# GpSimd fills in a pair's block sums before it halves the next pair's columns; one throwaway product; a later down matrix request

## The reference

```python
B, H, S, D = q.shape          # 4, 8, 768, 64
block, window = (32, 16)
nb = S // block               # 24
k_sum = k.reshape(B, H, nb, block, D).max(axis=3)
v_sum = v.reshape(B, H, nb, block, D).mean(axis=3)
scores_l = scale * np.matmul(q, k.transpose(0, 1, 3, 2))
mask_l = np.abs(pos[:, None] - pos[None, :]) < window
scores_s = scale * np.einsum('bhsd,bhnd->bhsn', q, k_sum) + np.log(block)
a = softmax(concat(where(mask_l, scores_l, -1e9), scores_s))
out = a @ concat(v, v_sum)
```

## Time and profile before

| | |
|---|---|
| median of 3 runs | 364.32 us (363.89, 364.32, 366.35) |
| the profiled execution | 365.38 us, of which its span is 363.5 us |
| PE busy | 326.4 us (90%), 3264 instructions |
| DVE busy | 172.5 us (47%) |
| ACT busy | 148.4 us (41%) |
| POOL busy | 101.0 us (28%) |
| DMA | 81.64 MB, 225 GB/s mean |
| mean granted TensorE clock | 0.974 |

### The profile page before, as it was taken

The page is one execution under the profiler, slowest core; times in us unless marked ns, Lnnn a source line. Parts: engine busy times, 40 slices in busy tenths (PEclk is TensorE's granted clock), DMA queues, the critical chain, the costliest instruction groups (busy, mean ns, idle before and its releaser), DMA issues.

```text
span 363.5 us, 9091 instructions
## 1 busy us (share of the span) xinstructions
PE 326.4 (90%) x3264; PEld 235.2 (65%) x3265; DVE 172.5 (47%) x391; ACT 148.4 (41%) x344; POOL 101.0 (28%) x181
## 2 busy tenths in 40 slices
PE   0869899999999899989867799999999999999993
PEld 0557677767666763323327248888888888888882
DVE  2546777878777562560114678423231323222331
ACT  1456778778778532221110073223132222313131
POOL 5466576676754300000000000222121212121211
PEclk9978999999999999999996799999999999999998
DMA  7999999999999996999950920110101101110101
GB/s 302 358 422 417 418 346 352 375 358 349 362 413 418 434 392 250 384 403 437 400 227 2 357 107 3 58 58 29 58 29 58 50 37 46 40 58 29 58 31 61
DMA packets 15147, 81.64 MB, mean 225 GB/s; under 512 B 2312, under 2 KB 2312, under 8 KB 10512
## 3 DMA queue, kind: packets, MB, share of 16 engines
q1 hardware_dynamic: 11936, 73.08, 50.7%
q0 software_dynamic: 1920, 6.29, 4.5%
q10 hardware_dynamic: 1264, 1.92, 1.6%
HBM read 74.99 MB, written 6.29 MB: 224 GB/s over the span
## 4 chain that ended last, share of the span: by engine, by line
PE 67%; DMA 11%; DVE 7%; ACT 7%; issue 4%; SPq 2%; POOL 1%; DVEq 0%; ACTq 0%; POOLq 0%
PE ps L923 35%; DMA ring<-in_moe_w 7%; PE ps L642 6%; DMA ring<-in_vt 4%; PE ps L619 3%; DVE ps L1187 3%; ACT work L990 3%; PE ps L655 3%; PE ps L909 3%; PE ps L628 2%; PE ps L761 2%; PE ps L611 2%; ACT work L1005 2%; SPq L296 2%; PE ps L810 2%
## 5 line engine op out<-in xcount | busy, mean ns | idle before, releaser
L923 PE MATMUL ps<-high_w2b,hid_high 128*128 (+1 forms) x184 | 71.7, 390 | 0.0
L923 PE MATMUL ps<-low_w2b,hid_high 128*128 (+1 forms) x184 | 71.7, 390 | 0.0
L923 PE MATMUL ps<-high_w2b,hid_low 128*128 (+1 forms) x184 | 71.6, 389 | 0.0
L990 ACT ACTIVATE work<-ps,small 128x120 f32<-128x120 f32 x192 | 53.6, 362 | 33.8 <-DVE small L1191 33.2
L576 POOL DMA_INDIRECT out_x<-work,small x24 | 23.6, 981 | 143.3 <-DVE small L1414 88.0
L1421 DVE SCALAR_TENSOR_TENSOR hid_low<-ps,hid_high 128x1024 fp32r<-128x1024 f32 x26 | 31.8, 1224 | 57.3 <-ACT hid_high L1102 57.2
L1084 ACT ACTIVATE work<-ps,small 128x512 f32<-128x512 f32 x24 | 16.5, 689 | 94.7 <-PE ps L923 87.8
L642 PE MATMUL ps<-ring,work 121*64 121x65 f32 x768 | 34.5, 232 | 8.8 <-ACT work L1005 4.0
L642 PEld LDWEIGHTS ps<-ring,work 121*64 121x64 f32 x768 | 27.8, 141 | 18.7 <-issue 11.3
L923 PEld LDWEIGHTS ps<-high_w2b,hid_low 128*128 128x128 f32 x184 | 34.6, 188 | 7.3
L923 PEld LDWEIGHTS ps<-high_w2b,hid_high 128*128 128x128 f32 x184 | 34.6, 188 | 6.8
(11 more groups left out here) (231 smaller groups left out, 363.6 us busy)
## 6 DMA issues: line engine op xcount, KB each, us to landing
ring<-in_moe_w SPq DMA_DIRECT2D x12, 2048.0 KB, 16.2
ring<-in_qk SPq DMA_DIRECT2D x16, 1104.0 KB, 8.5
ring<-in_v SPq DMA_DIRECT2D x16, 780.0 KB, 6.5
ring<-in_moe_w SPq DMA_DIRECT2D x10, 512.0 KB, 18.4
x_or_g<-in_moe_w SPq DMA_DIRECT2D x2, 2048.0 KB, 9.5
ring<-in_vt SPq DMA_DIRECT2D x7, 384.0 KB, 5.5
comb<-in_vt SPq DMA_DIRECT2D x7, 384.0 KB, 5.6
whole_w2b<-in_moe_w SPq DMA_DIRECT2D x4, 512.0 KB, 9.1
```

Of the source, the lines that this page charges most:

```text
L923: last = pe.matmul(ps[:, 4 + u, :], hidden_part[:, u, m * P:(m + 1) * P], matrix[:, bass.ds(e * UNIT + m * DM, DM)], start=m == 0 and i == ...
L990: act.activation(probs[u][:, j, :], sc[u][:, j // 2, (j % 2) * KC:(j % 2 + 1) * KC], ACT.Exp, bias=negmax[u][:, j:j + 1], scale=float(D) * ...
```

## The change

Three edits, and no transfer and no GpSimd instruction more or less:

```diff
@@ SP: request of the first expert's down matrix
             with sp.If(n_used < FEW + 1):
+                sp.wait_ge(w1b_part[0], 16)
                 for c in range(4):
@@ GpSimd: the loop over the pairs
             for n in range(1, B * NPAIR):
                 fill_gaps(n)
+                fill_sums(n)
                 if n + 1 < B * NPAIR:
                     halve(n + 1)
-                fill_sums(n)
@@ TensorE: the last round of the soft mixture's down product
                 for m in range(4):
                     if pr == E // 2 - 1 and m % 2 == 0:
+                        if m:
+                            keep_at_work(1, 1, comb[:, 0:BANK // SLOTS, :].rearrange("p q s -> p (q s)"))
                         for u in range(2):
                             pe.wait_ge(last_half[m // 2][u], 32)
```

## The result

| | before | changed |
|---|---|---|
| median | 364.11 us (4 runs) | 399.77 us (4 runs, 399.39 to 400.97) |
| ratio | | 1.0985, 95% interval 1.0947 to 1.1022 |
| span of the profiled execution | 363.5 us | 399.1 us |
| mean granted clock | 0.974 | 0.938 |

The account below looks back on a forecast made before the run. Attention was taken as bound by latency, a chain hopping between engines. Loop +31.0, clock +3.7, product -0.3 and request -0.4 make +34.0 us, taking the median 364.3 to 398.3 us; range 392 to 404.

Parts of the forecast that it names:

- The loop of 9.06 us, +31.0: Attention: the moved halving enters a loop of 9.06 us a pair against 6.41, paid over 14 turns, +31.0 us.
- The clock, +3.7: TensorE in attention: longer waits lower the clock in five of 14 turns, +3.7 us; bounds 0 to 10.4 us.
- two never follow each other: Attention: a slow pair leaves a shorter wait behind it, so two slow pairs in a row were not expected.
- After pair 15 nothing is moved.: From the last attention pair on, the new order was to add no time.
- The product, -0.3: Throwaway product in TensorE's 2.26 us wait for the last weights: fits for free, gains only by clock, -0.3 us.
- the request, -0.4: Down matrix requested after the up matrix's first part: gain at most 0.67 us, loss at most 1, taken as -0.4.
- Full clock with both small gains whole: Lower end of the prediction's own case: the loop without clock falls, product and request gains whole, 394.0 us.
- TensorE's fourteen waits behind pair 1: Sign in attention: TensorE waits for GpSimd ahead of each pair's first product, 14 times, over 30 us in all.
- R2: Later attention gives expert weights more time, winning back up to 25 us, down to 373 us; 4%.
- R1: Attention: the next pair's first product has time in hand, so the late halving is free, about 361 us; 3%.
- R3: The clock stays low throughout attention, making TensorE the bound: up to +84 us, 448 us; 3%.
- R4: Same loop in attention but the clock never falls: 394.6 us; 30% of the prediction's own 90% case.

Follow-up runs that it names:

- e1: The kernel before with GpSimd's new order alone, without the throwaway product and the later down matrix request: 399.87 us against 363.98, ratio 1.096.
- e5, e6: Label not tied in the text; apparently the changed kernel with either the halving's first addition left out (379.95 us) or gaps filled ahead of the halving (401.83 us).
- e12: Label not tied in the text; apparently the changed kernel with one extra 384-column addition in the halving: 413.84 us against 364.62, ratio 1.134.

## Why the prediction was right

Predicted 398.3 us, range 392 to 404; measured 399.8. The mechanism was right: the order alone is the loss, and the halving is what stands in the loop. By the prediction's steps, in the profiled execution:

- *The loop of 9.06 us, +31.0.* Measured 9.02 us a turn, 14 x 9.02 = 126.3 against 95.8: +30.4 us, less 0.1 as pair 1 started at 16.02. The six-product run confirms it apart from the clock, the longer and shorter halvings confirm what it is made of. Reading the new order's 5.02 us off the start of the old trace was what made this term exact; the rows after have 16.02 - 10.99 = 5.03 us there again.
- *The clock, +3.7.* The six long turns add 0.51, 0.72, 0.33, 0.74, 0.74 and 0.42 us, 3.5 in all. The number was a choice between bounds and its closeness is part luck: I had a fall cost 0.74 us or nothing, and took five turns. The clock fell in eight of the fourteen; six of them became longer, three of these by 0.7 us, and two kept 9.02 us (those from 34.57 and 99.49, where it fell about 1 us behind the first product). The thought that two never follow each other was wrong (turns 5 and 6, 12 and 13). The rule of the Trainium skill that I weighed, page "TensorE: Matmul & The Clock Gate", section "Why this matters for your kernels", would have given 394.6; the trace did not agree with it, as the clock fell behind waits of 2.51 to 2.71 us, and with the shorter halving behind 1.47 us. My own premise, that the length of the wait decides, does not hold either.
- *"After pair 15 nothing is moved."* This step failed. The last pair found the low clock (L594 at 145.75 takes 0.61 us) and had no wait of the loop behind it to hide in: from its first product to the end of the last weighted values it took 12.4 us, not 10.2, +2.3 us. The 2.3 us are this execution's, not the change's as such: in the profile of e1, whose median is the same, that stretch took 10.1 us at full clock, and in those of e5, e6 and e12 11.3 to 11.4.
- *The product, -0.3, and the request, -0.4.* Together -0.45 us in this pair of profiles, from the end of the last pair to the end of the program (399.1 - 158.2 = 240.9 us, before 363.5 - 122.1 = 241.4). That is inside the scatter of this stretch (239.7 to 243.7 us without the product), and e1, without either edit, has the median of the changed kernel to 0.1 us. So neither term is confirmed. The rows below, TensorE's, show where the three places went: the wait for the last weights fell from 2.26 to 1.43 us because the product, 1.12 us, now fills part of it, and the products on these weights began 66.6 us behind the end of the last pair, not 66.9; L843 took 2.28 us, so the clock fell all the same; L876 waited 1.99 us for the first part, 0.28 less, but then 1.09 us for a later one, 0.42 more than in the earlier trace rows.

```profile
222.25 1.12 PE L700 MATMUL ps<-comb,ident 128*128 128x512 f32 x2
224.80 1.92 PE L813 MATMUL ps<-ring,work 128*32 128x512 f32 x16 [1.43 <-DMA ring<-in_moe_w]
...
229.57 2.28 PE L843 MATMUL ps<-small,x_or_g 128*128 128x32 f32 x12 [0.31 <-DVE small L1333]
...
240.07 4.49 PE L876 MATMUL ps<-ring,soT 128*64 128x512 f32 x12 [1.99 <-DMA ring<-in_moe_w]
...
242.91 0.62 PEld L876 LDWEIGHTS ps<-ring,soT 128*64 128x64 f32 x4 [1.09 <-DMA ring<-in_moe_w]
```

The sum: 30.4 - 0.1 + 3.5 + 2.3 - 0.5 = 35.6 us, the difference of the spans; the forecast was 34.0. It came so near partly by luck, as a loop 0.7 us too long stands against the 2.3 us of the last pair.

Two smaller slips. Full clock with both small gains whole is 364.3 + 31.0 - 1.2 - 0.7 = 393.4 us, not the 394.0 of the prediction. And TensorE's fourteen waits behind pair 1 came to 27.5 us (28.8 - 1.3), not to over 30: where the low clock stretches a turn's products they fill part of the wait ahead of the next pair, of which 1.25 us were left at 43.59.

Of the rivals, R2 (the weights' stream hides part of it) is out, as the stretch behind attention kept its length to 0.5 us, and so are R1 and R3. R4, full clock, is what the six-product run made: 394.9 where I had 394.6.

## What to carry to other kernels

An engine's idle time takes work for nothing only if the work stands ahead of the wait that makes the idle time. Behind that wait, it lengthens any loop that needs its result. Ask of a moved step which loop it stands in, not how busy its engine is. Here 2.8 us of additions cost nothing ahead of a wait for another engine and 2.6 us a turn behind it, because the next turn's first product needs them. And look for a place in the old trace where the new order already stands: its rows give the new turn without any model.

## What the runs showed of the hardware

- The granted clock can fall after TensorE has gone back to work. In the kernel with the longer halving it fell about 1.6 us after the first product behind a wait of 2.68 us; there the fall was free, since only products with time to spare came after it. In the changed kernel it did so in two turns, which kept their 9.02 us. So how long the waits are does not tell what they cost; where in the turn the fall lands does.
- The lower level (1.2 GHz) made six of fourteen turns of the changed kernel longer, by 0.3 to 0.7 us: four behind waits of 2.51 to 2.71 us, two behind 1.87 and 1.91. With the longer halving it was two of fourteen, by 0.7 us and behind 3.62 us, though the mean granted clock there was lower (0.923 against 0.938). With the shorter halving the clock fell behind a wait of 1.47 us, and four of fourteen turns were 0.3 to 0.7 us longer.
- Six throwaway products, 1.5 us, in each wait kept the granted clock at 1.00 through the 127 us of attention, and left waits of 1.0 to 1.2 us.
- A throwaway product is cheap only if its price is read from the same kind: 0.245 us for an ordinary f32 product of 128x128, and 0.163 us for the f32 transposes that I had taken for the same.
